# A two-layer MLP stack behind linear attention: eight half-size block products per layer made seven, on tiles of 1024 tokens

## What is computed

```python
state = gamma * state + k_t v_t^T;  y_t = scale * q_t state      # 4 batches, 8 heads of 64, 768 steps
x = y laid out as (3072 tokens, 512)
h = np.maximum(x @ w_in, 0.0)                # w_in 512 x 2048
x = h * h @ w_mid                            # w_mid 2048 x 512
xn = x / sqrt(mean(x * x) + 1e-6) * rms_g
g, val = xn @ w_gate, xn @ w_val             # 512 x 1536 each
out = (silu(g) * val) @ w_out                # 1536 x 512
```

## Time and profile before

| what | us |
|---|---|
| median of 3 runs | 1223.78 |
| the 3 runs | 1223.75, 1223.78, 1223.80 |
| span of the profiled execution | 1221.4 |
| TensorE busy in it | 1210.5 |
| VectorE busy | 661.9 |
| ScalarE busy | 513.3 |
| GpSimd busy | 21.4 |

### The profile page before, as it was taken

How to read it: one execution, slowest core, us unless ns; L and a number is a source line. 1 busy time by engine, 2 the same in 40 slices (tenths; PEclk the granted TensorE clock), 3 DMA queues, 4 the chain that set the end, 5 groups by cost and what they waited for, 6 DMA issues and landing times.

```text
span 1221.4 us, 16292 instructions
## 1 busy us (share of the span) xinstructions
PE 1210.5 (99%) x5996; PEld 1005.4 (82%) x5996; DVE 661.9 (54%) x1017; ACT 513.3 (42%) x858; POOL 21.4 (2%) x24
## 2 busy tenths in 40 slices
PE   7999999999999999999999999999999999999998
PEld 6888888888888888888888888888888888888887
DVE  5665457664566445456545466444556544555433
ACT  1114445454445444344444344444354444344332
POOL 1220000000000000000000000000000000000000
PEclk9999999999999999999999999999999999999999
DMA  9986900000001000001000001000000000000000
GB/s 355 390 315 227 359 1 9 1 0 10 18 1 44 1 1 10 17 0 43 0 0 10 17 0 43 0 0 9 10 7 35 0 0 1 1 1 35 1 1 34
DMA packets 30869, 61.25 MB, mean 50 GB/s; under 512 B 2400, under 2 KB 12640, under 8 KB 30816
## 3 DMA queue, kind: packets, MB, share of 16 engines
q1 hardware_dynamic: 27936, 55.36, 12.5%
q10 hardware_dynamic: 2880, 5.24, 1.1%
HBM read 49.06 MB, written 11.53 MB: 50 GB/s over the span
## 4 chain that ended last, share of the span: by engine, by line
PE 99%; DMA 1%; DVE 0%; SPq 0%; ACT 0%; POOL 0%; issue 0%; ACTq 0%; POOLq 0%
PE bank L414 25%; PE bank L416 25%; PE bank L415 25%; PE bank L463 5%; PE bank L464 5%; PE bank L462 5%; PE bank L394 2%; PE bank L361 2%; PE bank L376 2%; PE bank L384 2%; DMA chunk<-qkv 1%; PE bank L480 0%; POOL k_dec L338 0%; SPq L260 0%; DVE hid_low L785 0%
## 5 line engine op out<-in xcount | busy, mean ns | idle before, releaser
L414 PE MATMUL bank<-xn_high,ring_high 128*128 128x512 f32 x576 | 226.1, 393 | 0.0
L416 PE MATMUL bank<-xn_high,ring_low 128*128 128x512 f32 x576 | 224.2, 389 | 0.0
L415 PE MATMUL bank<-xn_low,ring_high 128*128 128x512 f32 x576 | 224.2, 389 | 0.0
L781 DVE TENSOR_TENSOR pre<-pre,bank 128x512 f32<-128x512 f32 x72 | 49.5, 687 | 227.1 <-PE bank L416 227.1
L778 DVE TENSOR_TENSOR pre<-pre,bank 128x512 f32<-128x512 f32 x96 | 65.9, 686 | 169.3 <-ACT pre L574 169.3
L414 PE MATMUL bank<-x_high,ring_high 128*128 128x512 f32 x384 | 149.9, 390 | 0.0
L414 PE MATMUL bank<-hid_high,ring_high 128*128 128x512 f32 x384 | 149.5, 389 | 0.2 <-DVE hid_low L785 0.2
L415 PE MATMUL bank<-x_low,ring_high 128*128 128x512 f32 x384 | 149.4, 389 | 0.0
L416 PE MATMUL bank<-x_high,ring_low 128*128 128x512 f32 x384 | 149.4, 389 | 0.0
L415 PE MATMUL bank<-hid_low,ring_high 128*128 128x512 f32 x384 | 149.4, 389 | 0.0
L416 PE MATMUL bank<-hid_high,ring_low 128*128 128x512 f32 x384 | 149.4, 389 | 0.0
(11 more groups left out here) (66 smaller groups left out, 1545.4 us busy)
## 6 DMA issues: line engine op xcount, KB each, us to landing
chunk<-qkv SPq DMA_DIRECT2D x48, 512.0 KB, 8.7
out<-y_buf SPq DMA_DIRECT2D x24, 256.0 KB, 2.1
x_scratch<-y_sb ACTq DMA_DIRECT2D x20, 256.0 KB, 6.4
x_stage<-x_scratch SPq DMA_DIRECT2D x16, 256.0 KB, 2.8
w_gate_sb<-w_gate SPq DMA_DIRECT2D x1, 3072.0 KB, 13.9
w_val_sb<-w_val SPq DMA_DIRECT2D x1, 3072.0 KB, 20.0
w_out_sb<-w_out SPq DMA_DIRECT2D x1, 3072.0 KB, 27.2
w_in_sb<-w_in SPq DMA_DIRECT2D x1, 1792.0 KB, 12.9
```

The lines of the kernel that those rows point to most:

```text
L414: nc.tensor.matmul(dst, w_high, x_hi, start=start, stop=False)
L415: nc.tensor.matmul(dst, w_high, x_lo, start=False, stop=False)
L416: return nc.tensor.matmul(dst, w_low, x_hi, start=False, stop=stop)
L781: nc.vector.tensor_tensor(pre[:], pre[:], val_ps[:], ALU.mult).then_inc(hidden_ready, 1)
```

## The change

All four matmul layers are written as products of 2x2 blocks, and the eight block products of a layer are replaced by seven (Winograd's form of Strassen's method) with sums and differences of blocks as operands. The tokens are cut in 3 tiles of 1024, each in two halves of 512 (`N`).

- A front run makes two blocks of 128 hidden features by both halves of features and tokens: seven products of 12 matmuls of 512 columns (`front_run`). A tile has 4 front runs for the first MLP and 6 for the second, in all 30 in the kernel.
- A back run takes the layer out of the hidden features. For the first MLP it has 28 groups (seven products by `G1` = 4) of 12 matmuls of 512 columns. For the second it has 21 groups (`G2` = 3) of 24 matmuls of 256 columns, where the tokens are the stationary operand. There are 3 of each.
- The seven products of a run go to the PSUM pairs X, Z, Y, X, Y, Z, Y. In between, X is copied to Y (`seed`), and Z and Y are saved in SBUF (`save_p5`, `save_u2`), all three on ScalarE with 1024 columns. VectorE adds the saved parts to two of the four results.
- The hidden activations of a tile (`hid`, 64 KB in each partition) stay on chip, and the back run reads them in seven combinations. VectorE makes the combinations in place and the low part of each "hop", 128x1024; ScalarE makes its high part.
- The differences and sums of weight blocks (`sum_w`, `sum_back`) and the low parts of all weights (`low_w`, `low_back`) are made by GpSimd, 128x512 each; ScalarE makes the high parts (`high_w`, `high_back`). For the first tile GpSimd makes the low parts and combinations of x as well, beside attention, 128x1024 each.
- Weights are read from HBM again for each tile: 1 MB for a front run, and 36 or 27 blocks of 256 KB for a back run, through a ring of four.
- The norm of a tile is made in the first front run of the second MLP: the squares summed by 8 small float32 matmuls (`token_squares`), the root and reciprocal on 8 columns, and two float32 matmuls of 512 columns to spread it over the partitions (`spread`). PE waits for both.
- All loops are written out.

The core of the diff:

```diff
-T = 512
-TILES = B * S // T
+N = 512
+TILES = 3
+Q1, Q2 = 8, 6
+R1, R2 = Q1 // 2, Q2
+G1, G2 = Q1 // 2, Q2 // 2
+WR, HR, BR = 4, 3, 4
+A, Bb, C, Dd = range(4)
+OPERAND = (A, A, A, C, Bb, Dd, A)
```

On TensorE:

```diff
+            def banks_free(run, k):
+                if k == 0 and run:
+                    pe.wait_ge(x_taken, run)
...
+                if k == 2:
+                    pe.wait_ge(seeded, run + 1)
+                if k == 4:
+                    pe.wait_ge(u2_saved, run + 1)
+                if k == 5:
+                    pe.wait_ge(p5_saved, run + 1)
+                if k == 6:
+                    pe.wait_ge(c22_done, run + 1)
...
+            def front_run(run, m, fresh, front, norm=None):
+                for k in range(7):
+                    banks_free(run, k)
+                    if norm is not None and k == 2:
+                        token_squares(norm)
+                    if norm is not None and k == 4:
+                        spread(norm)
+                    pe.wait_ge(w_lo, 7 * m + k + 1)
+                    if fresh:
+                        pe.wait_ge(front_lo, 7 * front + k + 1)
+                    dst = (X, Z, Y, X, Y, Z, Y)[k]
+                    for u in range(2):
+                        cols = slice(u * P, u * P + P)
+                        for kb in range(2):
+                            mm = three(dst[:, u, :], w_ops[:, k, 0, kb, cols], w_ops[:, k, 1, kb, cols],
+                                       ops[:, k, 0, kb, :], ops[:, k, 1, kb, :], k < 2 and kb == 0)
+                    mm.then_inc(product_done, 1)
+
+            def back_run(bk):
+                for n in range(bk.groups):
...
+                    pe.wait_ge(hop_lo, bk.base + n + 1)
+                    pe.wait_ge(back_lo, bk.base + n + 1)
...
+                            for tb in range(4):
+                                rows = slice(tb * P, tb * P + P)
+                                place = dst[:, tb // 2, (tb % 2) * 2 * P:(tb % 2 + 1) * 2 * P]
+                                mm = nc.tensor.matmul(place, hop[:, 0, q, rows], slot[:, 0, q, :],
+                                                      start=first and tb % 2 == 0, stop=False, skip_group_check=True)
```

On VectorE and GpSimd in a back run, and the pace of each (`n` is the group that TensorE is about to do):

```diff
+            def low_hop(bk, n):
+                k, g = divmod(n, bk.ng)
+                hop = hop_at(n)
+                dve.wait_ge(hop_hi, bk.base + n + 1)
+                nc.vector.tensor_tensor(hop[:, 1], hid[:, 2 * g:2 * g + 2, OPERAND[k], :], f32(hop[:, 0]),
+                                        ALU.subtract).then_inc(hop_lo, 1)
+                if k > 3:
+                    return
+                a, b, c, d = (hid[:, 2 * g:2 * g + 2, s, :] for s in range(4))
...
+                if k == 0:
+                    dve.wait_ge(h_b, made)
+                    op = nc.vector.tensor_tensor(a, b, a, ALU.subtract)
...
+            def low_back(bk, n):
+                slot = wb_at(bk.w_slot(n))
+                pool.wait_ge(back_hi, bk.base + n + 1)
+                nc.gpsimd.tensor_tensor(slot[:, 1], back_source(bk, n), f32(slot[:, 0]),
+                                        ALU.subtract).then_inc(back_lo, 1)
...
+            def back_run(bk):
+                for n in range(bk.groups):
+                    if n + 4 < bk.groups:
+                        sum_back(bk, n + 4)
+                    if n + 3 < bk.groups:
+                        low_back(bk, n + 3)
```

More of the change, by code:

```diff
@@ L31 @@
 NCH = B * CH
-T = 512
-TILES = B * S // T
[L34 to L37, removed]
-EPS = 1e-6
[L43 to L62, removed]
@@ L65 @@
[L65 to L81, removed]
@@ L113 @@
[L113 to L118, removed]
+N = 512
+EPS = 1e-6
+TILES = 3
+Q1, Q2 = 8, 6
+R1, R2 = Q1 // 2, Q2
+RUNS = R1 + 1 + R2 + 1
+FR = R1 + R2
+G1, G2 = Q1 // 2, Q2 // 2
+GROUPS = 7 * (G1 + G2)
@@ L220, in build @@
-        QT, KT, K, V = range(4)
[L222 to L244, removed]
@@ L252, in build, with square_at, stored_chunks, x_place @@
+        def square_at(s):
+            return hid[:, 2 * s:2 * s + 2, C, :]
+        def stored_chunks():
+            return [(b, c) for b in range(B) for c in range(CH) if not (b < 2 and c < 4)]
+        def x_place(b, c):
+            if c < 4:
+                return b // 2, b % 2, c * P
+            return 2, b % 2, (b // 2) * 2 * P + (c - 4) * P
         block = ctx.enter_context(nc.Block())
@@ L380, in attend @@
                     pe.wait_ge(k_scaled, (CH - 1) * b + (c + 1))
-                    if c == 0 and not first:
+                    if c == 0 and b:
                         pe.wait_ge(state_ready, (CH - 1) * b)
@@ L469, in phase @@
-            def phase(ph):
-                for f, (_, i) in enumerate(ph.steps):
-                    front(ph, f)
-                    if i is not None:
-                        if f:
-                            back(ph, f, i, ph.kind, f - 1)
-                        else:
-                            back(ph, f, i, ph.before, BLOCKS[ph.before] - 1)
-                    if ph.before == MLP1 and f == SUM_AT:
-                        pe.wait_ge(squares, 7 * half(ph) + 7)
-                        nc.tensor.matmul(sum_ps[:], ones[:], rms[:], start=True, stop=True)\
-                            .then_inc(square_sum, 1)
@@ L483, in _ @@
[L483 to L492 removed]
+            scores(0)
+            for n in range(NCH):
+                if n + 1 < NCH:
+                    scores(n + 1)
+                attend(n)
@@ new lines, in _ @@
+            pe.wait_ge(w_lo, 1)
+            pe.wait_ge(front_lo, 1)
+            for u in range(2):
+                nc.tensor.matmul(Y[:, u, :], w_ops[:, 0, 0, 0, 0:P], ops[:, 0, 0, 0, :], start=True, stop=True,
+                                 skip_group_check=True)
+            for t in range(TILES):
+                for p in range(R1):
+                    front_run(run_f1(t, p), FR * t + p, p == 0, 2 * t)
+                back_run(BackRun(t, False))
+                for q in range(R2):
+                    front_run(run_f2(t, q), FR * t + R1 + q, q == 0, 2 * t + 1, t if q == 0 else None)
+                back_run(BackRun(t, True))
@@ L509, in copy_out @@
-                if not (isinstance(b, int) and b == 0):
-                    act.wait_ge(x_stored[c - 2 if c >= 2 else CH - 2 + c], 16 * b)
-            for c in range(CH):
-                copy_out(0, c)
-            with act.Fori(1, B - 1) as b:
-                for c in range(CH):
-                    copy_out(b, c)
-            stage = x_stage[:].rearrange("p n t -> p (n t)")
-            def split_x(src, k, loaded, count):
-                act.wait_ge(loaded, count)
-                nc.scalar.copy(x_high[:, k, :], src).then_inc(x_high_ready, 1)
@@ new lines, in seed, with save_p5, save_u2 @@
+            def seed(run):
+                act.wait_ge(*done(run, 0))
+                if run:
+                    act.wait_ge(y_taken, run)
+                nc.scalar.copy(Y[:], X[:]).then_inc(seeded, 1)
+            def save_p5(run):
+                act.wait_ge(*done(run, 1))
+                nc.scalar.copy(p5[:], Z[:]).then_inc(p5_saved, 1)
+            def save_u2(run):
+                if run == 0:
+                    for i in range(3):
+                        act.wait_ge(x_stored[i], 16 * len(stored_chunks()[i::3]))
+                act.wait_ge(*done(run, 2))
+                nc.scalar.copy(u2[:], Y[:]).then_inc(u2_saved, 1)
```

1318 lines of the change are left out of this document (856 added, 462 removed).

## The result

The change makes the kernel slower: 1323.19 us (median of 4 runs, 1322.01 to 1323.50) against 1223.76 on the same chip, a ratio of 1.081 with a 95% interval of 1.079 to 1.083. The forecast was 1211.4, and the range went from 1148 to 1265.

What follows compares the result with a forecast made beforehand. TensorE, busy 99%, was taken as the bound. Start 102.1, matmuls 800.5 and 181.4, end 4, norm 18 made 1106; exclusion with entries 99 and attention 4 made 1209, plus 2.4 gave 1211.4 us; range 1148 to 1265.

Steps and rivals of the forecast that it cites:

- The matmul stream: TensorE's matmuls in front and back runs: 982 us where it was 1111, so 129 us to be won.
- rival (c): Back runs: 256-column matmuls bound by stationary loads, or clock falling in waits; 1270 us; chance 0.05, other PE waits included.
- The serial account of VectorE and GpSimd: Back runs: instructions of both engines reading SBUF exclude each other, 1.08 plus 0.91 us a pair; 99 us with entries.
- Rival (b): Back runs: weaker exclusion, VectorE never waits for GpSimd; about 57 us in place of 99, 1170 in all; chance 0.21.
- its term for GpSimd: Back runs: a GpSimd instruction of 512 columns takes 1.04 us, counted as 0.91 in a serial pair.
- rival (a): Back runs: GpSimd's instruction dearer than 1.04 us (gain gone from 1.11) or hand-over losses; 1226 to 1268 us; chance 0.32.
- The entry of the back runs: Start of each back run: VectorE's leftover queue delays it, 2 us in the first MLP, 4 in the second.
- Attention: GpSimd's added x work in attention delays `scale_q` and `move_state`, for which TensorE waits: 4 us (0 to 8).
- The norm: PE waits for the norm's small matmuls, spread and late chain: 6.0 us a tile, 18 in all.

## Why the prediction was wrong

- **The matmul stream** was right to the tenth: 19.04 us a front run, and 256 columns at 0.120 between starts (from 1254.74 to 1256.42 in 14 steps, below). 129 us were there to be won, and rival (c) is excluded in its first form.

```profile
1254.74 0.28 PE L674 MATMUL Z<-ops 128*128 128x256 f32 x1
...
1256.42 0.28 PE L678 MATMUL Z<-ops 128*128 128x256 f32 x1
```

- **The serial account of VectorE and GpSimd** was right as a mechanism, and shown by the runs with PSUM input and with zeros. Rival (b) has fallen. Mis-sized was its term for GpSimd: 1.04 us for 512 columns. In this kernel k scaling still has a median of 1042 ns, and an instruction with two plain inputs has 1267 at the least and 1290 as the median:

```profile
L393 POOL TENSOR_TENSOR k_dec<-chunk,decay_k_sb x20: 1032/1042/1499, 11.4 to 116.7; 128x512 f32<-128x512 f32 x20
```

```profile
L421 POOL TENSOR_TENSOR w_ops<-sums_w,w_ops x120: 1267/1294/2292, 38.7 to 1213.5; 128x512 fp32r<-128x512 f32 x120
L421 POOL TENSOR_TENSOR w_ops<-raw_w,w_ops x90: 1275/1290/2266, 34.6 to 1217.4; 128x512 fp32r<-128x512 f32 x90
```

  Less the same start of 0.14, that is 1.13 in place of 0.91, and a heavy group is 2 x 1.08 + 2 x 1.13 = 4.42 (measured 4.45) in place of 3.97. In a back run of the first MLP this makes 10 x 0.45 + 4 x 0.23 + 6 x 0.45 = 8 us more, 101 in all. The one row there was had an operand broadcast over 64 columns, as rival (a) said; it was also a multiplication, where the new ones add and subtract, and no run separates the two. Rival (a) was right in kind: 1.27 is over its threshold of 1.11, and the change is slower even with attention in order (1302 us). Its upper bound, 1.24, was still too low, and its range ended at 1268. The Trainium skill, "GPSIMD Engine Reference", section 3.1, gives 4497 ns for an addition of 2048 columns, and a quarter of it, an estimate of 1.12 us, is too low here as well (1.27 measured). It did lie over the threshold of 1.11, and so pointed the right way.
- **The entry of the back runs** was sized too small in the first MLP and too large in the second. Its queue on VectorE was named and put at 2 and 4 us, which with the serial groups makes 5.97 and 7.97 us for the first group. From start to start it took 7.5 three times in the first MLP, and 7.3, 7.4 and 5.0 in the second. With every link longer by the exclusion TensorE waits 4.60 us after the first group, and then runs 8 matmuls at half its clock:

```profile
206.03 0.39 PE L596 MATMUL X<-ops 128*128 128x512 f32 x1
211.03 0.79 PE L594 MATMUL X<-ops 128*128 128x512 f32 x1 [4.60 <-DVE ops L1003]
211.62 0.63 PE L595 MATMUL X<-ops 128*128 128x512 f32 x1
212.04 0.63 PE L596 MATMUL X<-ops 128*128 128x512 f32 x1
...
214.25 1.21 DVE L1003 TENSOR_TENSOR ops<-hid,ops 128x1024 fp32r<-128x1024 f32 x1
...
215.51 0.50 PE L594 MATMUL X<-ops 128*128 128x512 f32 x1
```

  From start to start these take 0.43 us where 0.227 is usual: 8 x 0.2 = 1.6 us. Hardly any of it is lost: VectorE's low part for the next group ends at 215.46 and the group starts at 215.51, so TensorE would have had to wait for it at full clock too. At the six entries the group behind the slow matmuls starts 0.05 to 0.1 us after VectorE's low part, except at one, where it is 0.4 us. Rival (c) had dismissed a fall of the clock with waits of 1.3 us; it hadn't counted the entries. The mean granted clock of the run is 0.963.
- **Attention** was the step that failed outright: put at 4 us (0 to 8), it was 25. The prediction asked which instructions exclude each other, and not what is queued behind a wait. `sum_w(0, 0)` waits for a DMA that SP issues behind twelve transfers of q, k and v, and `low_x(0)` for a cast two chunks ahead; both stand in front of k scalings. At most 3 of the 25 us were exclusion or the length of the work: the run with the new order starts at 105.2, within the forecast's 106.
- **The norm** was put at 6 us and cost 11 to 12. TensorE's own part was 4.8 to 5.4 us, not 3.7 (its 16 records took 2.9 to 3.6, the spread 1.9). The rest is a wait of 4.35 us for the squares (the row names no releaser; VectorE's last sum ended at 319.32), with two of VectorE's sums lasting 2.29 and 1.64 in place of 1.22 and 0.69 beside GpSimd, and the slow clock after it, which made product 2 last 4.9 to 5.2 us in place of 2.7:

```profile
315.35 2.29 DVE L1052 TENSOR_TENSOR hid<-hid 128x1024 f32<-128x1024 f32 x1
317.68 1.64 DVE L1055 TENSOR_TENSOR hid<-hid 128x512 f32<-128x512 f32 x1
...
319.42 2.91 PE L622 MATMUL R<-ones,hid 128*128 128x2 f32 x16 [4.35 <-issue]
...
328.41 1.29 DVE L1075 TENSOR_TENSOR gt<-eye_sb,rinv_t 128x512 f32<-128x512 f32 x2
...
329.99 1.88 PE L630 MATMUL R<-gt,ones 128*128 128x512 f32 x4
```

  The slow clock is in large part hidden here as well: VectorE has the diagonal ready at 329.70 and the spread starts at 329.99 (0.3 us later; 1.1 and 0.8 in the other tiles), so a faster product 2 would most likely have met a wait for the diagonal, as the run with the norm later did. That the chain as a whole is late is shown by the run that moved it; how much each link has of it was not taken apart.

Of the 112 us that the forecast missed, 21 are attention's order, 18 the norm, and 74 the back runs. Some 42 of those 74 are GpSimd's dearer instruction: 8 us in each of the first MLP's back runs by the sum above, and about 6 in the second's by the same steps. The other 32 are read off the distances from group to group alone. They aren't at the entries, whose surplus in the first MLP (1.5 us each) and shortfall in the second (0.7, 0.6, 3.0) cancel. In the first MLP's back runs groups 8 and 9 (counted from 0) take 4.4 to 4.5 us, where the sum had 3.06, and groups 20 and 21, with the next front's work, 4.4 and 3.5, where it had 2.72. In the second's, groups 5 to 7 take 4.4 to 4.5 in place of 3.06, and group 11 takes 8.9 in the first two tiles in place of 6.13. Why groups with only one GpSimd instruction in the sum kept the pace of the heavy ones was not taken apart by a run, and that part of the cause stays open.

The forecast gain was 12 us. Attention's order, the norm, or the dearer GpSimd instruction would each have taken it away alone.

## What to carry over

Two engines that wait for each other, as VectorE and GpSimd do here, are one engine in the sum: add their times before asking whether the work fits, and ask whether the faster one should do all of it. VectorE alone was 84 us faster than both together. A price for such an instruction must come from the same operation on the same kind of operands. When work is put into an in-order queue beside something urgent, look at what it waits for before looking at how long it takes. And matmuls at half the clock cost only what the wait behind them doesn't hide.

## What the runs showed of the hardware

Undisturbed, GpSimd's subtraction or addition of 128x512 float32 took 1.27 us with two plain inputs, and its multiplication 1.04 us with one input broadcast along 64 columns; 1024 columns, plain, took 2.34 to 2.36. A VectorE instruction with both inputs in SBUF and a GpSimd instruction that reads SBUF waited for each other in both orders, VectorE's 1.21 becoming 2.30 us. With one VectorE input in PSUM, or beside a GpSimd memset of 0.53 us, VectorE's took 1.22 us. The granted clock was half after a wait of 4.6 us on TensorE, for 8 matmuls, and stayed full through the waits of 1.3 to 1.5 us before the groups that followed.
